# Routing the first block of rows from one batch while the second is in attention, with the means of v added up by GpSimd

## The reference

```python
k_sum = k.reshape(B, H, nb, 32, D).max(axis=3)
v_sum = v.reshape(B, H, nb, 32, D).mean(axis=3)       # 24 means of 32 rows each
mask_l = np.abs(pos[:, None] - pos[None, :]) < 16
a = softmax(concat(scale * q @ k.T under mask_l, scale * q @ k_sum.T + log(32)))
x = (a @ concat(v, v_sum)).transpose(0, 2, 1, 3).reshape(1536, 512)

logits = x @ w_gate                                   # 1536 x 8
expert_idx = np.argmax(logits, axis=1)
for e in range(8):                                    # w1[e]: 512x1024, w2[e]: 1024x512
    rows = expert_idx == e
    out[rows] = gate_w[rows, None] * (np.maximum(x[rows] @ w1[e], 0) @ w2[e])

h = out @ w_in                                        # w_in: 512x2048, w_out: 2048x512
result = np.maximum(0.01 * h, h) @ w_out
```

## Time and profile before

| | us |
|---|---|
| median of 3 runs | 573.67 (572.54 to 574.70) |
| the profiled execution, whole | 574.64 |
| its span, first to last instruction | 572.9 |
| attention, start to the last product with v | 103.3 |
| from there to block 0's first product | 29.1 |
| the four blocks | 157.6 |
| from there to the last stage's first product | 12.1 |
| the last stage | 270.7 |

### The profile page before, as it was taken

How to read it: one execution, slowest core, us unless ns; L and a number is a source line. 1 busy time by engine, 2 the same in 40 slices (tenths; PEclk the granted TensorE clock), 3 DMA queues, 4 the chain that set the end, 5 groups by cost and what they waited for, 6 DMA issues and landing times.

```text
span 572.9 us, 9201 instructions
## 1 busy us (share of the span) xinstructions
PE 529.8 (92%) x3162; PEld 430.9 (75%) x3163; DVE 281.1 (49%) x535; ACT 255.6 (45%) x539; POOL 64.3 (11%) x102
## 2 busy tenths in 40 slices
PE   3799999349999999989979999999999999999997
PEld 2377577347888888968867888888888888888885
DVE  2567477545442543765205723753642763642631
ACT  4478487314443343664304634641543550553520
POOL 5310240053013103230210000000000000000000
PEclk9989999667999999999997999999999999999999
DMA  9999361068246244580442064052254041340001
GB/s 209 225 203 243 83 163 50 37 204 298 87 166 217 57 165 166 183 290 7 177 158 100 1 220 148 1 185 98 85 220 146 0 165 56 145 146 0 0 18 55
DMA packets 76682, 74.16 MB, mean 129 GB/s; under 512 B 45424, under 2 KB 49520, under 8 KB 76656
## 3 DMA queue, kind: packets, MB, share of 16 engines
q1 hardware_dynamic: 72368, 62.28, 36.2%
q0 software_dynamic: 2560, 8.39, 4.6%
q10 hardware_dynamic: 1728, 3.15, 1.6%
HBM read 63.32 MB, written 10.49 MB: 129 GB/s over the span
## 4 chain that ended last, share of the span: by engine, by line
PE 84%; SPq 4%; ACT 3%; DMA 3%; issue 3%; DVE 2%; POOL 1%; POOLq 0%; ACTq 0%; DVEq 0%
PE psum L1140 12%; PE psum L1141 12%; PE psum L1142 12%; PE psum L1156 12%; PE psum L1154 12%; PE psum L1155 12%; PE psum L1020 2%; PE psum L1053 2%; ACT p_sb L567 2%; PE psum L1036 2%; PE psum L1109 1%; PE psum L1011 1%; SPq L303 1%; PE psum L995 1%; PE psum L982 1%
## 5 line engine op out<-in xcount | busy, mean ns | idle before, releaser
L1140 PE MATMUL psum<-xT_hi,w_hi 128*128 128x512 f32 (+1 forms) x320 | 123.2, 385 | 3.8 <-DVE w_lo L872 2.3
L1141 PE MATMUL psum<-xT_lo,w_hi 128*128 128x512 f32 (+1 forms) x320 | 122.5, 383 | 0.0
L1142 PE MATMUL psum<-xT_hi,w_lo 128*128 128x512 f32 (+1 forms) x320 | 122.3, 382 | 0.0
L1154 PE MATMUL psum<-w_hi,h_hi 128*128 128x512 f32 x296 | 115.9, 392 | 0.0
L1156 PE MATMUL psum<-w_hi,h_lo 128*128 128x512 f32 x296 | 115.2, 389 | 0.0
L1155 PE MATMUL psum<-w_lo,h_hi 128*128 128x512 f32 x296 | 115.2, 389 | 0.0
L872 DVE TENSOR_TENSOR w_lo<-w_raw,w_hi 128x512 fp32r<-128x512 f32 x80 | 51.4, 686 | 60.7 <-ACT w_hi L624 60.7
L1140 PEld LDWEIGHTS psum<-xT_hi,w_hi 128*128 128x128 f32 x320 | 61.1, 191 | 16.3 <-DVE xT_lo L882 4.8
L1142 PEld LDWEIGHTS psum<-xT_hi,w_lo 128*128 128x128 f32 x320 | 61.1, 191 | 11.7
L1141 PEld LDWEIGHTS psum<-xT_lo,w_hi 128*128 128x128 f32 x320 | 61.2, 191 | 11.4
L644 ACT ACTIVATE h_small<-psum 128x512 f32<-128x512 f32 x48 | 28.7, 598 | 90.3 <-PE psum L1142 90.3
(11 more groups left out here) (127 smaller groups left out, 510.6 us busy)
## 6 DMA issues: line engine op xcount, KB each, us to landing
w_raw<-in_moe_w_in SPq DMA_DIRECT2D x12, 1024.0 KB
w_raw<-in_moe_w_out SPq DMA_DIRECT2D x6, 2048.0 KB, 8.4
w_raw<-in_moe_w SPq DMA_DIRECT2D x8, 1024.0 KB
w_raw<-in_moe_w SPq DMA_DIRECT2D x4, 2048.0 KB, 9.1
vw<-in_v SPq DMA_DIRECT2D x20, 192.0 KB, 4.9
k_nat<-in_k SPq DMA_DIRECT2D x12, 256.0 KB, 5.0
q_nat<-in_q SPq DMA_DIRECT2D x12, 256.0 KB, 5.1
v_nat<-in_v SPq DMA_DIRECT2D x4, 768.0 KB, 7.6
```

What stands on the lines that cost most here:

```text
L1140: mm(h, w1_hi[:, c, cols], xT_hi[:, c, 0:n], start=(c == 0), stop=False)
L1141: mm(h, w1_hi[:, c, cols], xT_lo[:, c, 0:n], start=False, stop=False)
L1142: last = mm(h, w1_lo[:, c, cols], xT_hi[:, c, 0:n], start=False, stop=(c == KD - 1))
L1154: mm(y_ps[s % 2], h_hi[:, c, rows], w2_hi[:, c, :], start=(c == 0), stop=False)
```

## The change

- Only rows of batch 0 are routed to block 0, during steps 14 to 20 of attention: it takes the expert with most rows in batch 0, and of that expert's rows of batch 0 up to 512. Everything else (the rest of batch 0, and batch 1) is routed while block 0 is being computed, into blocks 1 and up. `n_blocks` is 1 plus the blocks of 512 that what is left of each expert needs.
- Block 0 is written out ahead of the loop, always at 512 columns and 4 tiles. Its w1 is loaded during attention, five of its eight splits stand in steps 19 to 23, and its gather and transposes stand before `weighted_v(23)` and behind it. The last tile's `transpose_x` and `gate_logits`, the counts (with more matmuls in place of VectorE's running sums) and the inversion stand between block 0's products.
- The buffers are laid out anew by hand, so that block 0's w1 and rows can lie where batch 0's k, v and the like were.
- `K_STEP` is 2. The means of v of batch 1 come from a copy of v with 8 rows on each of 96 partitions, which GpSimd halves three times (2048, 1024 and 512 elements a partition) before one product on TensorE in step 10.
- The 10 filler products and the zeroing of the banks go.

```diff
-K_STEP = 1
-V_STEP = K_STEP + PIECES
+K_STEP = 2
+MEAN_STEP = K_STEP + PIECES
+ROUTE_STEP = 14
+W1_STEP = UNITS - 5
...
+            def add_v_rows():
+
+                pool.wait_ge(v_rows_loaded, 16)
+                n, done = V_ROWS // 2, 0
+                while n:
+                    nc.gpsimd.tensor_tensor(v_rows[:, :, 0:n * D], v_rows[:, :, 0:n * D], v_rows[:, :, n * D:2 * n * D],
+                                            ALU.add).then_inc(rows_added, 1)
...
+            def mean_second():
+                pe.wait_ge(avg_ready, 2)
+                pe.wait_ge(ksum_maxed, 2 * B * PAIRS)
+                pe.wait_ge(q_ready, 2 + MEAN_STEP // 2)
+                pe.wait_ge(rows_added, 3)
+                mm(vsum_ps, avg_rows[:], v_rows[:, :, 0:D], start=True, stop=True).then_inc(vsum_done, 1)
...
+            def rank_first():
+
+                pe.wait_ge(routing_consts, 1)
+                pe.wait_ge(chosen_ready, 1)
+                for d in range(QT):
+                    mm(route_ps[:, d:QT, :], (ones if d else upper)[:], chosen[:, 0:QT - d, :], start=(d == 0), stop=(d == QT - 1))
+                for t in range(QT):
+                    last = mm(route_ps[:, QT, :], ones[:], chosen[:, t, :], start=(t == 0), stop=(t == QT - 1))
...
             for n in range(UNITS):            # VectorE
...
+                if n == ROUTE_STEP:
+                    choose(0)
+                if n == ROUTE_STEP + 2:
+                    first_expert()
+                    first_slots()
+                if n == ROUTE_STEP + 3:
+                    slot_parts(QT)
+                    hot_tiles(QT, SUB)
+                    hot_rows(QT)
+                if n == ROUTE_STEP + 4:
+                    chain(tt(chosen[:, 0:QT, :], chosen[:, 0:QT, :], left[:].unsqueeze(2).to_broadcast([P, QT, E]), ALU.mult))
+                    keep_gates(0)
+                if n == ROUTE_STEP + 6:
+                    tables(0, SUB)
+                if n >= W1_STEP:
+                    split_w1(0, n - W1_STEP)
...
             def weighted_v(n):                # TensorE
...
+                if n == ROUTE_STEP + 1:
+                    rank_first()
+                if n == ROUTE_STEP + 5:
+                    pe.wait_ge(hot_row_ready, 1)
+                    pe.wait_ge(hot_tile_ready, 2)
+                    invert(first_inv_ps, QT, SUB)
...
+                if n == UNITS - 1:
+                    transpose_first(0, 2)
+                weighted_v(n)
+            transpose_first(2, KD)
...
+            hidden(0, 0, 0)
+            transpose_x(T - 1)
+            hidden(0, 0, 1)
+            gate_logits(T - 1)
+            hidden(0, 0, 2)
+            pe.wait_ge(logits_ready, T)
+            hidden(0, 0, 3)
+            pe.wait_ge(chosen_ready, 2)
+            for t in range(T):
+                last = mm(total_ps, chosen[:, t, :], ones[:], start=(t == 0), stop=(t == T - 1))
+            last.then_inc(totals_done, 1)
+            hidden(0, 0, 4)
+            pe.wait_ge(blocks_ready, 1)
+            for d in range(T):
+                mm(place_ps[:, d:T, :], (ones if d else upper)[:], chosen[:, 0:T - d, :], start=(d == 0), stop=False)
+            mm(place_ps, blocks[:], start_rows[:], start=False, stop=True)
+            mm(ends_ps[:, 0, :], blocks[:, 0:1], up_to[:], start=True, stop=True).then_inc(places_done, 1)
+            for f in range(5, KF):
+                hidden(0, 0, f)
+            second_product(0, 0, 1)
+            pe.wait_ge(hot_row_ready, 2)
+            pe.wait_ge(hot_tile_ready, 4)
+            invert(inv_ps, T, LATER_TILES)
+            second_product(0, 1, 3)
+            transpose_rows(1, rows_gathered, 2, 0, 2)
+            second_part(0, 3, 0, KF // 2)
+            transpose_rows(1, rows_gathered, 2, 2, KD)
+            second_part(0, 3, KF // 2, KF)
...
-            with pe.Fori(0, MAXB) as j:
+            with pe.Fori(1, MAXB) as j:
```

More of the change, by code:

```diff
@@ L49 @@
 COLS = NSUM + BAND
+V_ROWS = 8
+V_PARTS = S // V_ROWS
 TOK = B * S
@@ L100, in build @@
+        spare = keep("spare", [P, LATER_TILES])
+        filled = keep("filled", [1, LATER_TILES])
+        used_f = keep("used_f", [1, MAXB - 1, 1])
+        ends = keep("ends", [1, 1, E])
+        behind = keep("behind", [1, MAXB - 1, E])
+        expert_f = keep("expert_f", [1, MAXB - 1, 1])
+        shared_from = kept[0]
+        att, att_end = region(shared_from)
+        q_nat = att("q_nat", [P, QT, H, D])
+        vsum = att("vsum", [NSUM, B, H, D])
         ksum_one = att("ksum_one", [P, B * PAIRS, NSUM])
-        kw = att("kw", [P, PAIRS, B, STRIPS, COLS])
@@ L805, in _ @@
-            before = count_sum[src][:, T_PAD - 1:T_PAD - 1 + T, :]
-            total = count_sum[src][:, T_PAD + T - 1, :]
-            tt(place[:], rank_ps, before, ALU.add).then_inc(route_step, 1)
-            step[0] += 1
-            blocks = block_sum[0][:, 0, E_PAD:]
-            chain(ts_(blocks, total, 0.0, None, ALU.is_gt))
-            for full in range(ROWS, TOK, ROWS):
-                chain(nc.vector.scalar_tensor_tensor(out=blocks, in0=total, scalar=float(full),
-                                                     in1=blocks, op0=ALU.is_gt, op1=ALU.add))
@@ new lines, in count_blocks @@
+            def count_blocks():
+                dve.wait_ge(totals_done, 1)
+                chain(ts_(blocks_some[:], total_ps, 0.0, None, ALU.is_gt))
+                for i in range(1, FULL_BLOCKS):
+                    last = stt(out=blocks[:] if i == FULL_BLOCKS - 1 else blocks_some[:], in0=total_ps,
+                               scalar=float(i * ROWS), in1=blocks_some[:], op0=ALU.is_gt, op1=ALU.add)
+                    if i < FULL_BLOCKS - 1:
+                        chain(last)
+                last.then_inc(blocks_ready, 1)
@@ new lines, in _ @@
+            dve.wait_ge(zeros_ready, 10)
+            for m in range(PIECES):
+                sum_k(m)
+            dve.wait_ge(mask_ready, 1)
+            softmax(0)
+            softmax(1)
+            copy_vsum(0)
+            spread_first()
+            for n in range(UNITS):
+                t, g = divmod(n, 2)
+                if g == 0 and t >= 2:
+                    keep_logits(t - 2)
+                if n >= 1:
+                    normalise(n - 1)
+                if K_STEP <= n < MEAN_STEP:
+                    sum_k(PIECES + n - K_STEP)
+                if n + 2 < UNITS:
+                    softmax(n + 2)
+                if n == MEAN_STEP:
+                    copy_vsum(1)
+                if n == ROUTE_STEP:
[12 more added lines that the diff above has]
+                    tables(0, SUB)
+                if n >= W1_STEP:
+                    split_w1(0, n - W1_STEP)
```

870 lines of the change are left out of this document (487 added, 383 removed).

## The result

The changed kernel takes 591.30 us (median of 585.37, 591.09, 591.50 and 593.46) beside 573.11 of the kernel before on the same chip: a ratio of 1.0284 with an interval of 1.024 to 1.0328. Forecast were 576.3 and a range up to 583. The change is slower, on the side that had the largest chance, but by 18 us and not by 3. The profiled execution is the slowest of the four, 593.46 us with a span of 591.7.

The account below looks back on a forecast made before the run. TensorE was taken as the bound, with the stretch from attention's last product to block 0 left to win. Block 0 ending 20.8 us earlier and a fifth block's +23.4 gave +2.6 on 573.7: 576.3 us, range 571 to 583.

Parts of the forecast that it names:

- The adds: GpSimd's three additions for the mean of v in attention: 7.4 us, done by 54, before TensorE wants them about 57.
- rival 3: GpSimd's adds take 17.7 us, so TensorE stands 4 to 7 us in step 10: 580 to 583 us, chance 0.05.
- rank_first, the inversion: In attention, 12 + 12 small bf16 matmuls on a TensorE without slack, 0.99 us per twelve: +2.0 us.
- VectorE's routing: In steps 14 to 18, some 25 short operations push normalise and weighted_v: +1.0 us, bounds 0 and 2.4.
- the splits: In steps 19 to 23, VectorE's split_w1 waits for ScalarE's split and delays normalise: +1.5 us, 0 to 3.5.
- `K_STEP`: Early attention: wait for k gone, -1.3 us; clock fall at 27 to 34 us perhaps gone, -1.5 (none to 3.0 saved).
- the means: In attention, TensorE's matmuls for the mean of v and a wait for q's copy go, less one call: -5.4 us.
- TensorE's wait for the gathered rows: Before block 0: TensorE reaches transpose_first at 99.0, rows come at 101.7, a wait of 2.7 us.
- Block 0: First matmul at 104.1, 28.4 us earlier; length 54.8 us; ends at 158.9 against 179.7, a gain of 20.8.
- Rival 1: Shorter waits, full clock near 30 us and at block 0, successor's rows in time: 571.2 us; chance with milder forms 0.42.
- The fifth block: Expert stage, one more small block: 17.0 for its matmuls, 1.8 for transposes, 4.6 before the last stage, +23.4 us.
- The pace: Time per 512-column matmul, taken as 0.227 us from the kernel before; the sum had no term for a change.

Follow-up runs that it names:

- the layout as before: The changed kernel with the expert stage's buffers back at 32 over a multiple of 512 bytes: 579.68 us, ratio 1.0075 to the kernel before.
- the run of its own: The kernel before made to run five blocks instead of four, the fifth a small one: 598.84 us, ratio 1.0425.
- both repairs: The changed kernel with expert-stage buffers at 32 over a multiple of 512 bytes and the second mean of v on TensorE: 576.93 us, ratio 1.0083.
- the means alone: The changed kernel with the second batch's mean of v taken by TensorE instead of GpSimd's additions: 586.91 us, ratio 1.0212.
- `K_STEP` alone: The kernel before with `K_STEP` 2 instead of 1 and all six products of the second mean of v in step 10: 571.25 us, ratio 0.9933.

## Why the prediction was wrong

**The adds, "Hidden".** This step failed, in two ways. The price was right (7.4 us forecast, 8.3 found), but not the time: v_rows landed 13.2 us behind its issue at 38.5, not 9.1 behind 37, so the additions began at 51.79 and not at 46. They ended at 60.10, and TensorE reaches this product at 56.45 in the kernel without them.

The other harm the sum did not look for at all; rival 3 doubted the additions only for their own length. It lies in VectorE's operations: in four cases (56.34 and 56.50, 56.05 and 56.22, 59.82 and 59.98, 56.23 and 56.40) a copy within SBUF ends 0.16 to 0.17 us behind the addition that was running. The sentence "VectorE's long operations in steps 3 to 9 read PSUM" passed over a short one, the copy of `ksum_one`, that reads and writes SBUF; an operation's own length says nothing of what it can lose by waiting. The operations beside it that reduce within SBUF (0.65 us) were not held. The Trainium skill (SBUF — State Buffer, "Who interferes with whom") has this as a lock: a copy on VectorE can run in a mode that takes the pair of ports it shares with GpSimd, and whichever of the two comes second "fully blocks"; the four pairs of ends agree. The prediction took the additions' price from the skill and left this out.

In the changed kernel the two ways cover each other: with a free copy the product would still have had to wait for additions that ended some 3.6 us too late. With the layout as before the copies alone did it: TensorE stood 3.29 us in step 9, and the product waited for nothing. Against their absence the additions cost 5.8 us up to step 12 (4.4 + 1.4) and 8.6 up to step 23, where the sum had hidden work. The device times are less clear: taking them out gave 4.1 us, with intervals that touch, and nothing by the ratios where the layout was already repaired.

**Attention otherwise.** The total was right, in part by luck. For rank_first, the inversion, VectorE's routing and the splits the sum had 2.0 + 1.0 + 1.5 = 4.5 us to step 23; the runs show 4.5, up to 1 us of it from the clock. But the 24 small products cost 0.6 and not 2.0: their price, 0.99 us for twelve, was read where the granted clock was 0.50. VectorE's routing cost 1.9 and not 1.0, and steps 20 to 22 gave 2.0 and not 1.5. `K_STEP` took the better end of its bounds: the clock stayed at 1.00, and step 3 comes 4.6 us earlier, 1.8 more than I took; the means gave 4.8 instead of 5.4. TensorE's wait for the gathered rows, forecast 2.7, is 2.77, but behind it the clock was 0.57, and that stretch cost 1.5 more. With 0.2 of a later start, 8.6 - 1.4 + 0.9 + 0.5 - 1.8 + 0.6 + 1.5 + 0.2 is the +9.1 of the first row of the table.

**Block 0.** 50.4 instead of 54.8. The clock was 1.00 from its first product (1.8 in the sum; in two of the four changed kernels it was 0.82 over the first 4 us), and TensorE shows no wait for block 1's rows (1.8 in the sum). Rival 1 had this right, and its gain was covered by the adds. Its 50 small products took 2.2 us and not 4.1, priced by the same row at half clock, and the pace put 1.2 on top: 54.8 - 1.8 - 1.8 - 1.9 + 1.2 = 50.5.

**The fifth block.** 23.4 in the sum, 23.1 by the trace of the run of its own, and 25.8 (21 to 28) by the medians. The mechanism and the size were right; it is what makes the change slower whatever else is repaired. In the changed kernel with both repairs the stretch from block 0's end to the last stage takes 148.3 us where the sum had 145.9: the old small block takes 22.6 instead of 21.3, the new one with the step to the last stage 1.2 more than the sum had.

**The pace.** This step failed too, and it is the largest miss: no term of the sum at all. I took (45.2 - 1.7) / 192 = 0.227 from a kernel whose buffers lie level and used it for one whose buffers I knew to be "laid out anew". The range for that was zero. It cost 7.4 us in the last stage and, at the same 0.0064, 2.8 in blocks 1 to 4 (432 long products) and 1.2 in block 0, 11.4 in all; the 192 short products were not slower (0.118 to 0.119 us each, 0.120 before). It is also what put the time outside the range: with the layout alone repaired the kernel takes 579.68 us, with the means alone 586.91.

Of the signs that the prediction named, the 40 relus, the 304 groups, the 16.8 us to the last stage and the wait of 2.77 us for the gather came. Block 0's first matmul came at 113.2 and not near 104, and mean_second waited 0.50 us.

With both repaired the changed kernel takes 576.9 us. For that version the sum would have been 576.3 + 4.4 for TensorE's five products, 580.7: 3.8 too much. In its trace block 0 is 4.9 shorter than in the sum, the last stage, which began at full clock, 2.1 shorter, and blocks 1 to 4 are 2.4 longer; so part of this nearness is chance.

What stays open: whether the two repairs' gains add in time (the ratios do not tell), whether the second fall of the clock hangs on the additions, and why TensorE slows down when the stationary and the moving operand are not level. That hi against lo matters on its own was not tried apart from a difference to the stationary side.

## What to carry to other kernels

Before work is put on GpSimd because that engine is idle, list what VectorE copies within SBUF at that time and who waits behind those copies: each can be held to the end of the GpSimd operation that it meets. Ask also when the work's inputs land: here the additions were over 3.6 us too late even for a kernel that nothing held. When buffers are laid out by hand, keep all operands of one product at the same distance from a multiple of 256 bytes, and compare the pace of the plain matmuls first. And where a split of work depends on how rows fall into fixed blocks, count the blocks before pricing anything else; here one more cost 23 us, and the hidden routing brought block 0 forward by 20.1 (84.84 us behind step 0 with both repairs, 104.95 with `K_STEP` alone).

## What the runs showed of the hardware

- 512-column products of float32r, high and low parts, run at 0.2271 us each when stationary and moving operands lie level modulo 256 bytes in a partition, and at 0.2335 to 0.2337 when one of them is 96 or 128 bytes off, 2.8% slower. Shifts of all by 64 or 320 bytes, or of one side by 256 or 512, change nothing. Products of 256 columns show no such loss. I had expected no such dependence.
- A copy of 128 x 288 float32 numbers within SBUF on VectorE takes 0.31 us, and 0.81 to 3.78 when it meets a two-input addition running on GpSimd, ending 0.16 to 0.17 us behind it.
- The load of the same 1.5 MB of v landed 13.2 us behind its issue in both runs that put 8 rows on each of 96 partitions, and after 8.7 and 9.7 us in the two that put 6 on each of 128.
- A short stop of TensorE reached much further than itself: behind waits of 2.54 and 0.50 us its clock was 0.67 from 60 to 67 us, where the same kernel without the additions had 1.00. Behind a wait of 1.86 us it was 0.54 and 0.68 from 88 to 98 us in two kernels and 1.00 in two others; what decides is not shown.
- Small products of the identity in TensorE's waits kept its clock at 1.00 into block 0 (128 to 132 us: 18 matmuls instead of 11 in 4 us).
